# Two more weight pieces rounded ahead of the first gates, the second tile's input split on VectorE, two layer-2 pieces swapped, one dummy matmul pair added

## The reference, cut to what matters

```python
x = conv(x)                       # out[s] = sum_k w[h, k] * x_pad[s + k], w = softmax(weight)
h = x @ w_in;  g = h * np.cos(h);                     x = g @ w_out      # layer 1
h = x @ w_in2; g = h * np.clip(h + 3.0, 0, 6) / 6.0;  y = g @ w_out2     # layer 2
```

## Time and profile before

| what | value |
|---|---|
| time, median of 3 runs | 2242.18 us (2240.41 to 2242.32) |
| the profiled execution | 2241.01 us, of which the span is 2239.3 us |
| PE matmul busy | 2224.8 us, 99% of the span |
| DVE, ACT, POOL busy | 1820.3, 1737.1, 1509.4 us (81, 78, 67%) |
| mean granted TensorE clock | 0.999 |

### The profile page before, as it was taken

How to read it: one execution, slowest core, us unless ns; L and a number is a source line. 1 busy time by engine, 2 the same in 40 slices (tenths; PEclk the granted TensorE clock), 3 DMA queues, 4 the chain that set the end, 5 groups by cost and what they waited for, 6 DMA issues and landing times.

```text
span 2239.3 us, 56917 instructions
## 1 busy us (share of the span) xinstructions
PE 2224.8 (99%) x19484; PEld 1835.3 (82%) x19484; DVE 1820.3 (81%) x2498; ACT 1737.1 (78%) x2847; POOL 1509.4 (67%) x1070
## 2 busy tenths in 40 slices
PE   9999999999999999999999999999999999999999
PEld 6788888888888888888888888888888888888887
DVE  8778888888888888888888888888888888888754
ACT  7787777887777877778777788777787777877775
POOL 7876666666666666666666666666666666666664
PEclk9999999999999999999999999999999999999999
DMA  4110000000000000000000000000000000000001
GB/s 106 41 23 16 15 1 13 14 14 14 9 5 14 14 14 14 0 14 14 14 14 1 13 14 14 14 9 5 14 14 14 14 0 14 14 14 7 4 6 23
DMA packets 208860, 33.14 MB, mean 15 GB/s; under 512 B 203184, under 2 KB 207280, under 8 KB 208816
## 3 DMA queue, kind: packets, MB, share of 16 engines
q1 hardware_dynamic: 205648, 32.14, 8.1%
q10 hardware_dynamic: 3168, 0.39, 0.1%
HBM read 19.92 MB, written 12.58 MB: 15 GB/s over the span
## 4 chain that ended last, share of the span: by engine, by line
PE 96%; POOL 2%; ACT 1%; DVE 1%; issue 1%; POOLq 0%; DVEq 0%; ACTq 0%
PE h_ps L473 45%; PE acc L480 30%; PE acc_tail L487 20%; POOL g_lo L1184 1%; PE acc_tail L724 0%; POOL wout L1195 0%; ACT g_hi L768 0%; ACT pre L754 0%; DVE gate L942 0%; ACT pre L764 0%; POOL wtail_lo L1204 0%; POOL wtail_lo L1202 0%; PE h_ps L716 0%; DVE halo L1008 0%; DVE xT_tail L1007 0%
## 5 line engine op out<-in xcount | busy, mean ns | idle before, releaser
L1184 POOL TENSOR_TENSOR g_lo<-gate,g_hi 128x512 fp32r<-128x512 f32 x1024 | 1469.4, 1456 | 702.7 <-ACT g_hi L768 701.9
L480 PE MATMUL acc<-g_hi,wout 64*128 64x512 f32 x4096 | 1417.6, 386 | 4.0 <-POOL wout L1195 4.0
L480 PEld LDWEIGHTS acc<-g_hi,wout 64*128 64x128 f32 x4096 | 754.1, 184 | 84.5 <-POOL wout L1195 5.3
L473 PE MATMUL h_ps<-in_hi,win_hi 64*128 64x512 f32 x2048 | 791.1, 387 | 2.9 <-POOL wtail_lo L1204 1.5
L487 PE MATMUL acc_tail<-g_lo,wout 64*128 64x512 f32 x2048 | 791.2, 386 | 0.0
L487 PE MATMUL acc_tail<-g_hi,wout 64*128 64x512 f32 x2048 | 791.1, 386 | 0.0
L480 PE MATMUL acc<-g_lo,wout 64*128 64x512 f32 x2048 | 790.9, 386 | 0.0
L473 PE MATMUL h_ps<-in_tail,wtail_hi 64*128 64x512 f32 x2048 | 790.4, 386 | 0.3
L473 PE MATMUL h_ps<-in_lo,win_hi 64*128 64x512 f32 x2048 | 790.2, 386 | 0.0
L473 PE MATMUL h_ps<-in_hi,win_lo 64*128 64x512 f32 x2048 | 789.5, 386 | 0.0
L768 ACT ACTIVATE g_hi<-gate 128x512 fp32r<-128x512 f32 x1024 | 624.3, 631 | 110.5 <-DVE gate L945 51.2
(11 more groups left out here) (114 smaller groups left out, 2329.0 us busy)
## 6 DMA issues: line engine op xcount, KB each, us to landing
out_dram<-o_blk SPq DMA_DIRECT2D x128, 64.0 KB, 1.8
x_in<-in_x SPq DMA_DIRECT2D x126, 64.0 KB, 2.2
blk_tail<-in_x SPq DMA_DIRECT2D x62, 64.0 KB, 2.3
out_dram<-blk_tail SPq DMA_DIRECT2D x62, 64.0 KB, 1.8
stage<-in_moe_w_out SPq DMA_DIRECT2D x7, 384.0 KB, 3.4
stage<-in_moe_w_in SPq DMA_DIRECT2D x6, 256.0 KB, 3.7
stage<-in_moe_w_in SPq DMA_DIRECT2D x2, 512.0 KB, 3.6
pre<-in_moe_w_in SPq DMA_DIRECT2D x2, 256.0 KB, 4.7
```

The costliest lines, as they stand in the source:

```text
L473: return pe.matmul(chunk_of(h_ps, q, half), w, x, start=start, stop=stop)
L480: return pe.matmul(acc[pair][:, :], wout[layer][rows, 2 * q + half, cols], g[rows, :], start=start, stop=stop)
L1184: pool.tensor_tensor(chunk_of(g_lo, q, half), chunk_of(gate, q, half), chunk_of(g_hi, q, half).bitcast(F32), ALU.subtract).then_inc(glo_re ...
```

## The change

It makes five edits. Ahead of phase 0 ACT rounds piece 5 as well as 4, and takes piece 6 between slot 0's copies and sines (`HIGH_BETWEEN` 5 to 6, `LOW_FIRST` 6 to 7); DVE's piece 7 goes to slot 0, and POOL takes 7, 8, 9 one slot earlier. In layer 2 the first quarter of `w_out` is now piece 15 (rounded by DVE in slot 15) and the tail rows of `w_in` are piece 16. In phase 1 the high parts of tile 0's drained result are made by DVE instead of ACT, its low tail goes from slot 14 to slot 15, the halo copies go from DVE to ACT, and one tap goes to slot 12. At the start, DVE takes tile 0's low tail ahead of the turn of tile 1, and TensorE gets one dummy pair between the two small matmuls that spread the taps.

```diff
+WARM_BETWEEN = 1
-                  Piece(1, IN, W, FF, 4, 0, 6), Piece(1, IN_TAIL, W, FF, 3, 0, 5)]
-        PIECES += [Piece(1, OUT, n * QUARTER, (n + 1) * QUARTER, 4 - n % 2, 0, 6 - n % 2) for n in range(4)]
+                  Piece(1, IN, W, FF, 4, 0, 6), Piece(1, OUT, 0, QUARTER, 3, 0, 5),
+                  Piece(1, IN_TAIL, W, FF, 4, 0, 6), Piece(1, OUT, QUARTER, 2 * QUARTER, 3, 0, 5),
+                  Piece(1, OUT, 2 * QUARTER, 3 * QUARTER, 4, 0, 6), Piece(1, OUT, 3 * QUARTER, CHUNKS, 3, 0, 5)]
...
-        HIGH_BETWEEN = 5
+        HIGH_BETWEEN = 6
-        LOW_FIRST, LOW_GATE = 6, 5
+        LOW_FIRST, LOW_GATE = 7, 5
...
-        THIRD_BY_ACT = {2: 0, 7: 1}
+        HALO_SECOND, THIRD_BY_ACT = 1, {2: 0, 5: 1}
-        CONV_SECOND = [2, 2, 2, 2, 2, 2, 2, 2, 4]
+        CONV_SECOND = [2, 2, 2, 2, 2, 3, 3, 3, 4]
-        LOW_TAIL_AT = {"drained": 6, "handed": 1}
-        SPLIT_DRAINED, TAIL_DRAINED, TWIN_DRAINED = 4, 5, 6
+        LOW_TAIL_AT = {"drained": 7, "handed": 1}
+        SPLIT_DRAINED, TAIL_DRAINED = 4, 6
...
                           stop=True).then_inc(taps_spread, 1)
+                ones_times_ones(WARM_BETWEEN)
                 pe.matmul(h_ps[:, 0, 0:TAPS], head_of[:, 0:P], w_soft[:, :], start=True,
                           stop=True).then_inc(taps_spread, 1)
...
                     if ph.setup == 1:
-                        if q == SPLIT_DRAINED:
-                            act.wait_ge(acc_read, ph.number)
-                            split_hi(in_f[L2][:, :], L2)
-                        if q == TAIL_DRAINED:
-                            split_tail(in_ftail[L2][:, :], L2)
-                        if q == TWIN_DRAINED:
-                            split_twin(in_ftail[L2][:, :], L2)
+                        if q == HALO_SECOND:
+                            put_halo(ph.convolved)
...
-            weight_high(4)
+            for n in (4, 5):
+                weight_high(n)
...
+            def split_high_drained(q):
+
+                if q == SPLIT_DRAINED:
+                    dve.wait_ge(acc_read, 1)
+                    dve.tensor_copy(in_hi[L2][:, :], in_f[L2][:, :]).then_inc(hi_ready[L2], 1)
+                if q == TAIL_DRAINED:
+                    dve.tensor_copy(in_tail[L2][0:DT, :], in_ftail[L2][:, :]).then_inc(hi_ready[L2], 1)
+                    dve.tensor_copy(in_twin[L2][DT:P, :], in_ftail[L2][:, :]).then_inc(twin_ready[L2], 1)
```

More of the change, by code:

```diff
@@ L275, in parts_of @@
                 (src[:, :, P:D], dst[:, :, P:D], dst[:, :, D:D + DT])]
[L277 to L280, removed]
-        HIGH_BETWEEN = 5
+        FIRST_PIECE_OF = {0: {2: 3, 4: 6, 6: 9}, 2: {0: 13, 4: 16}}
+        OUT_PIECES = {0: [4, 7, 10, 11], 2: [15, 17, 18, 19]}
+        HIGH_BY_DVE = {0: {0: 7, 2: 8, 3: 9, 5: 10, 6: 11}, 1: {0: 12, 1: 13, 2: 14, 7: 15}}
+        HIGH_IN = {2: {0: 16, 3: 17, 4: 18, 6: 19}}
+        HIGH_BETWEEN = 6
         BY_DVE = [n for at in HIGH_BY_DVE.values() for n in at.values()]
         BY_ACT = [n for n in range(len(PIECES)) if n not in BY_DVE]
-        LOW_FIRST, LOW_GATE = 6, 5
-        LOW_IN = {1: 6, 2: 7, 3: 8, 4: 9, 5: 10, 7: 11, 8: 12, 10: 13, 12: 14, 16: 15, 17: 16, 19: 17, 20: 18, 22: 19}
+        LOW_FIRST, LOW_GATE = 7, 5
+        LOW_IN = {1: 7, 2: 8, 3: 9, 5: 10, 7: 11, 8: 12, 10: 13, 12: 14, 15: 15, 17: 16, 19: 17, 20: 18, 22: 19}
         MAIN, TAIL = 0, 1
@@ L297, in conv_moe_kernel @@
         CONV_FIRST = [2, 2, 3, 4, 5, 6, 7, 7, 7]
-        CONV_SECOND = [2, 2, 2, 2, 2, 2, 2, 2, 4]
+        CONV_SECOND = [2, 2, 2, 2, 2, 3, 3, 3, 4]
         CONV_THIRD = [4, 6, 8, 10, 12, 14, 14, 14, 14]
-        HALO_SECOND = 1
         CONV = {0: [0, 0, 0, 1, 1, 1, 2, 3, 4], 1: [4, 6, 8, 10, 11, 14, 14, 14, 14]}
@@ L812, in keep_tail_halos, with put_halo @@
                                    ACT.Copy).then_inc(halo_ready, 1)
+            def put_halo(i):
+                act.wait_ge(x_turned, i + 1)
+                act.wait_ge(x_tail_turned, i + 1)
+                for buf, kept in ((xT, halo), (xT_tail[0:DT, :], halo_tail)):
+                    act.activation(buf[:, 0:HALO], halo_at(kept, i), ACT.Copy).then_inc(halo_ready, 1)
+                    act.activation(halo_at(kept, i + B), buf[:, TOK:], ACT.Copy).then_inc(halo_ready, 1)
             def tap_third(n):
@@ L1097, in phase @@
                     if ph.convolved is not None:
-                        if ph.layer == L1 and ph.setup != 0 and q == (HALO_SECOND if ph.setup == 1 else 0):
+                        if ph.layer == L1 and ph.setup not in (0, 1) and q == 0:
                             put_halo(ph.convolved)
@@ L1108, in phase @@
                         split_low_1(q)
+                    if ph.setup == 1:
+                        split_high_drained(q)
                     if q == DRAIN_SLOT and ph.before is not None:
@@ L1158, in _ @@
             split_low_first()
+            split_low_tail(acc_tail[1][0:DT, :], L2, 0)
             dve.wait_ge(halo_ready, 5)
             turn_main(1)
-            split_low_tail(acc_tail[1][0:DT, :], L2, 0)
             for t in range(CONV_BEFORE):
```

## The result

The changed kernel takes 2245.27 us (median of 19 runs, 2244.38 to 2246.56) where the kernel before takes 2240.54 us (19 runs beside it, 2238.97 to 2242.53): ratio 1.002, interval 1.0013 to 1.0027. It is slower by 4.7 us (2.9 to 6.0 by the interval), or 0.21%. That is just over the 4.5 us that I had called the least that can be told, and not the 0.75 us of my sum. The profiled execution of the changed kernel took 2245.11 us with a span of 2243.4 us, 4.1 us more than the span before.

The account below looks back on a forecast made before the run. PE was taken as busy throughout the loop, so only its earlier waits and clock loss, 8.9 us, could move. Terms summed to +0.75 us on 2241.01 us, giving 2241.8; 1.2 us for the median made 2242.9 us, range 2239.2 to 2246.6.

Parts of the forecast that it names:

- Phase 0, net 0: Slots 6 and 7: slot 6's 1.61 us wait goes, slot 7's grows from 0.75 to about 2.36 us; net 0.
- Rival 1: Phase 0 waits really go because POOL, not DVE, sets slot 7; 2.36 us less, 2240.5 us; chance 0.12.
- rival 4: Before slot 0: piece 5 lands late and ACT, waiting in order, delays slot 0; 2247 us; chance 0.02.
- Rival 2: Slots 6, 7, 16, 19 and the clock lose nothing, low tail in time; -8.6 us, 2233.6 us; chance 0.02.
- The start, -0.3: Ahead of slot 0: dummy pair raises the clock sooner or pushes taps back; middle taken, 0.3 us earlier.
- Slot 16, +4.2: Slot 16 waits for the low tail behind slot 15's gates, starting at 88.2 instead of 84.00; +4.2 us.
- the sentence on phase 1: Phase 1: PE does not wait for ACT or DVE, so the moved roundings and halo copies cost nothing by themselves.
- The clock at slot 16, +1.7: About 5 us idle ahead of slot 16 makes it start at the lower clock; +1.7 us, bounds 0 and 3.7.
- rival 3: Longer waits at slots 7 and 16 both cost clock, 3.7 us lost each; +6.45 us, 2248.6 us; chance 0.04.
- Slot 19 and its clock, -4.85: Swapped pieces remove slot 19's wait for a `w_out` piece, -3.15 us, and the lower clock behind it, -1.7 us.
- Slot 21, 0: Slot 21's 0.59 us wait for a piece that ACT rounds behind slot 19's gates stays; 0.

Follow-up runs that it names:

- the swap alone: Kernel before with only pieces 15 and 16 swapped (first quarter of layer 2's `w_out` rounded by DVE in slot 15); 2238.70 us, ratio 0.9992.

## Why the prediction was right or wrong

The time came out 2.4 us above the forecast, inside the range (2239.2 to 2246.6). That is in part luck: I had added 1.2 us because the median of three runs of the kernel before was 2242.18 us, and over 19 runs it is 2240.54. As a change the sum said +0.75 us, and the two spans say +4.1 and the medians +4.7, which is slower by just over the 0.2% for which I had a chance of 0.05. The path was right, and two terms were mis-sized.

- *Phase 0, net 0.* Right in every step, and shown twice: by slot 7's row in the changed kernel and in the one with pieces 5 and 6 ahead alone. Rival 1 fell; moving DVE's rounding removed the wait that POOL is named for. Piece 5 was hidden (rival 4 fell). Rival 2 fell too: slots 7 and 16 waited.
- *The start, -0.3.* Wrong in size and sign: +0.72 in the profile. "I take the middle" between a gain and a loss was the faulty step: there was no row for a gain. The pair's place in PE's order costs 0.37 us, beyond the 0.2 that I had as the bound, where the dummy pair is shown as 0.79 us long, not the 0.5 that I took. The rest is within the spread of the eight passes. That these passes are slow because of the clock is itself not shown: I had read it from their pace, 0.87 us each before 9 us and 2.74 / 6 = 0.46 behind it, but the granted clock reads 1.00 there (kernel before, L724 alone: us, then PE, PEld, clock, DMA):

```profile
5.00:9.00 4.00, 3.46 (x4) 1.52 (x5) 1.00 0.87 233
```

- *Slot 16, +4.2.* The mechanism was right (low tail behind gates, tap and rounding, the short low tail ahead of POOL, nothing behind 101 us), the size wrong: +6.6. The failed step is the sentence on phase 1, "PE does not wait for ACT or DVE there, so none of it counts by itself". PE doesn't, but the low tail stands on DVE, and DVE's delays of phase 1 arrive there: slot 15's gates ended at 89.36 us instead of 86.87. With the roundings back on ACT and the tap in slot 15 the delay is gone: the gates end within 0.3 us of where the prediction put them. In the same step I priced the roundings at 0.4 to 0.7 us and the moved tap not at all; the roundings took 1.51, 0.41 and 1.44 us and the tap 2.56. The Trainium skill ("SBUF — State Buffer", "Who interferes with whom") has not only the two-input rule that I quoted but, in the next lines, that a VectorE copy or cast in a two-port mode takes the shared pair as well. The casts above at 2.31, 1.51 and 1.44 us, and the six-column copies at 1.34, agree with it. I had read the rule and applied it to one instruction.
- *The clock at slot 16, +1.7.* Right, 1.9 by the sum above. The five kernels that waited there lost 1.6 to 2.7 us, near that or more but less than rival 3's 3.7, and slot 7's wait cost no clock.
- *Slot 19 and its clock, -4.85.* Right in the changed kernel, where slot 16 is late; with the swap alone and slot 16 in time only 2.3 us of it were left.
- *Slot 21, 0.* Right there too (-0.2), and +0.9 where slot 16 is in time.

The profiled execution is 0.5 us above the median of before and 0.2 below that of after; that gives the 4.7 us of the medians against 4.1 of the spans.

What stays open: how much the dummy pair does to the length of the first eight passes (by the estimate above, anything from -0.3 to +0.7 us would fit), and why the kernels that wait at slot 19 have single times some 3 us apart (2.9 to 3.9 with 10 to 19 runs, and 0.7 to 2.4 for all others). The stretch of low clock began together with the work in one profile and 1.4 us behind it in another, so the loss may differ from run to run; that was seen, not tested.

## What to carry to other kernels

A table of moved work has to be priced with what runs on the neighbouring engine at that moment: here a copy of six columns on DVE took 1.34 us beside POOL's work, more than the 0.75 us of an undisturbed 128x512 tap. When a wait is removed, follow the engine that releases it through the next two or three slots, since here each of three removed waits came back, wholly or in part, at a later step that the same engine serves (slot 6's at slot 7, slot 7's at slot 8, and with the swap alone slot 19's at slots 18, 20 and 21). And a step moved to an engine that "nothing waits for" counts as soon as the last step ahead of a phase is put behind it on that engine.

## What the runs showed of the hardware

- In the rows read here a DVE cast, copy or tap from SBUF to SBUF that begins while POOL is in a two-input low part ends within 0.6 us after POOL's instruction: a cast of 2.31 us and a tap of 2.56 us under the 2.40 of piece 14, and 1.34 us for 128x6 columns where ACT takes 0.19 for the same. The gates, one of whose inputs is in PSUM, take 1.30 us for two whether POOL works or not.
- PE idle for 2.1 us (slot 7) kept the clock at 1.00, that is at 2.4 GHz, in all six kernels with that wait; idle for 3.2 us (slot 19) it fell to 1.2 GHz in all five profiles that have the wait, in two of them only 0.8 and 1.4 us after work had begun again; idle for 3.9 to 6.9 us (slot 16) it fell in all five, in four of them while PE was still idle. A longer wait did not cost more clock: 6.9 us idle lost 1.9, 6.2 us idle 2.4.
- Ahead of slot 0 the same eight matmuls took 5.16 to 6.67 us in fourteen profiles, and two that are the same up to slot 15 (before and the swap alone) differ by 1.3 us. An early difference of a microsecond between two single profiles says nothing about the change.
